# The attention stage of a one-core kernel: output gate through a sigmoid, a reciprocal of eight numbers, heads in two halves of the rows, weight splitting moved from GpSimd to ScalarE and VectorE

## The reference

```python
for t in range(S):                       # S = 768, B = 4, H = 8, D = 40
    m_new = np.maximum(f_gate[:, :, t] + m, i_gate[:, :, t])
    f_stab = np.exp(f_gate[:, :, t] + m - m_new)
    i_stab = np.exp(i_gate[:, :, t] - m_new)
    C = f_stab * C + i_stab * np.einsum('bhd,bhe->bhde', vt, kt)
    n = f_stab * n + i_stab * kt
    h_tilde = np.einsum('bhde,bhe->bhd', C, qt)
    denom = np.maximum(np.abs(nq), 1.0)  # nq = n . q
    o = 1.0 / (1.0 + np.exp(-o_gate[:, :, t]))
    y[:, :, t] = o * h_tilde / denom
...
x = experts(x, w_gate, w1, w2)           # each token to one expert, relu between w1 and w2
return (x @ w_a) * (x @ w_b) @ w_out     # w_a, w_b: 320 x 1536
```

## Time and profile before

| | |
|---|---|
| median of three runs | 985.36 us (981.37 to 985.89) |
| the profiled execution | 981.72 us, of which 980.0 us are the span |
| attention, first `prob` to last `prob` | 28.37 to 195.76 us |
| of which tiles 3 to 23 | 54.74 to 195.76 us |
| first instruction of `experts` | 209.80 us |
| mean granted TensorE clock | 0.949 |

### The profile page before, as it was taken

How to read it: one execution, slowest core, us unless ns; L and a number is a source line. 1 busy time by engine, 2 the same in 40 slices (tenths; PEclk the granted TensorE clock), 3 DMA queues, 4 the chain that set the end, 5 groups by cost and what they waited for, 6 DMA issues and landing times.

```text
span 980.0 us, 17872 instructions
## 1 busy us (share of the span) xinstructions
PE 854.5 (87%) x6122; PEld 809.0 (83%) x6122; DVE 650.0 (66%) x1639; ACT 257.3 (26%) x493; POOL 187.9 (19%) x218
## 2 busy tenths in 40 slices
PE   1899999943479979998999899899989998999995
PEld 1899899932378979997898799789978988998995
DVE  7489999975756775577558656855775575265222
ACT  5222222200223331232124123312331242233221
POOL 7466767710100110011001100110110011011001
PEclk9989999965689999999999999999999999999998
DMA  3866667200321220041013001200310040032000
GB/s 88 225 170 186 191 186 212 88 13 11 98 71 41 69 77 14 2 119 41 0 31 107 20 0 59 79 20 0 103 56 0 2 135 21 1 93 67 1 1 21
DMA packets 49722, 66.59 MB, mean 68 GB/s; under 512 B 6592, under 2 KB 43984, under 8 KB 48720
## 3 DMA queue, kind: packets, MB, share of 16 engines
q1 hardware_dynamic: 43856, 54.25, 19.4%
q0 software_dynamic: 2368, 7.88, 2.8%
q10 hardware_dynamic: 3456, 3.93, 1.2%
HBM read 57.88 MB, written 8.16 MB: 67 GB/s over the span
## 4 chain that ended last, share of the span: by engine, by line
PE 46%; DVE 20%; issue 5%; ACT 4%; DMA 1%; POOL 1%; DVEq 0%; ACTq 0%; POOLq 0%
PE psA L875 17%; PE acc L898 11%; PE psB L875 8%; PE acc L923 6%; DVE at_slot L1241 2%; DVE ab L1327 2%; DVE w_lo L1265 2%; ACT ab_hi L1075 2%; DVE w_lo L1261 2%; PE psT L935 2%; DMA xg<-xs_dram,idx_g 1%; DVE w_hi L1263 1%; DVE cmp L1103 1%; PE psT L949 1%; PE psT L943 1%
## 5 line engine op out<-in xcount | busy, mean ns | idle before, releaser
L875 PE MATMUL psA<-x_hi,wa 128*128 128x384 f32 x480 | 135.5, 347 | 0.4 <-DVE x_lo L1353 0.4
L875 PE MATMUL psB<-x_hi,wb 128*128 128x384 f32 x480 | 132.3, 341 | 0.0
L840 POOL DMA_INDIRECT xg<-xs_dram,idx_g x24 | 25.6, 1068 | 499.2 <-DVE idx_g L1255 494.3
L875 PE MATMUL psB<-x_lo,wb 128*128 128x384 f32 x288 | 97.0, 337 | 0.0
L875 PE MATMUL psA<-x_lo,wa 128*128 128x384 f32 x288 | 96.9, 336 | 0.0
L1080 ACT COPY a_sb<-psA 128x384 f32<-128x384 f32 x96 | 46.1, 480 | 188.8 <-PE psB L875 188.7
L923 PE MATMUL acc<-wo_hi,ab_hi 128*128 128x320 f32 x288 | 91.9, 319 | 1.0 <-DVE ab_lo L1331 1.0
L923 PE MATMUL acc<-wo_lo,ab_hi 128*128 128x320 f32 x288 | 88.8, 308 | 0.0
L923 PE MATMUL acc<-wo_hi,ab_lo 128*128 128x320 f32 x288 | 88.7, 308 | 0.0
L1331 DVE TENSOR_TENSOR ab_lo<-ab,ab_hi 128x384 fp32r<-128x384 f32 x96 | 53.5, 558 | 52.3 <-ACT ab_hi L1075 52.1
L1327 DVE TENSOR_TENSOR ab<-a_sb,psB 128x384 f32<-128x384 f32 x96 | 52.9, 551 | 52.4 <-ACT a_sb L1080 52.1
(11 more groups left out here) (233 smaller groups left out, 1917.3 us busy)
## 6 DMA issues: line engine op xcount, KB each, us to landing
toks<-in_tok_dram SPq DMA_DIRECT2D x24, 484.0 KB, 5.1
w_raw<-in_w_dram SPq DMA_DIRECT2D x32, 320.0 KB, 3.2
w_raw<-in_w_dram SPq DMA_DIRECT2D x32, 256.0 KB, 3.0
qks<-in_qk_dram SPq DMA_DIRECT2D x24, 320.0 KB
w_raw<-in_w_dram SPq DMA_DIRECT2D x64, 64.0 KB, 2.8
xs_dram<-y ACTq DMA_DIRECT2D x24, 160.0 KB, 3.8
qst<-in_qk_dram SPq DMA_DIRECT2D x48, 60.0 KB
piece<-in_w_a_dram SPq DMA_DIRECT2D x6, 256.0 KB, 2.7
```

The source lines that it names most:

```text
L840: pool.indirect_dma_start(out=xg[:, t, 0:DM], out_offset=None, in_=xrows, in_offset=bass.IndirectOffsetOnAxis(ap=idx_g[:, t:t + 1], axis=0 ...
L875: last = pe.matmul(ps, w, x, start=(n == 0), stop=(n == len(steps) - 1))
```

## The change

1. The gate. `o_gate` is no longer a part of each tile's `toks`; one DMA per chunk (`load_gates`) brings it for four tiles into `gate`, and ACT turns it into a sigmoid in place (`open_gates`, 128x1280), one chunk ahead, in tile 3 of the chunk. Exp and Sigmoid are in different ACT tables, so a table load stands ahead of the sigmoid, and a one-number Exp (`reload`) with another table load behind it. The `ez` of each tile is gone.
2. The reciprocal. DVE takes it of `den` (128x8) right behind `den`. `normalize` multiplies `num` with it (128x320), `finish` multiplies with the gate (128x320).
3. Row halves. Heads 0 to 3 are in partitions 0 to 39, heads 4 to 7 in partitions 64 to 103 of `qks`, `arow` and `mrow`, and `exponents` and `scores` take them in turn: each product is over 40 partitions at 0 or at 64. The `qks` loads are two DMAs rather than one, the `arow`/`mrow` loads four rather than two. `exponents` stands directly behind `scores`, ahead of `transposes`.
4. `transposes` and `logits` take three full blocks of 128 (`y` has 64 more columns, zero).
5. The splitting. `w_a` and `w_b` have loads, semaphores and splits of their own: `load_piece(c, 0)` in SP's queue behind tile 1, `load_piece(c, 1)` behind tile 3. ACT makes the high part (`split_high`, one 128x768 copy) in tiles 0 and 2, DVE the low parts (`split_low`, 128x512 and 64x256) in tiles 1 and 3. POOL has no part in it any more.
6. ACT no longer zeroes `qks` at the start; POOL's memsets have half the columns, and there are eight of six partitions rather than four.

```diff
     def _(sp):
+        def load_gates(c):
+            sp.dma_start(gate[:, bass.ds(c, 1), :, :].rearrange("p c b n -> p (c b) n"),
+                         tok[bass.ds(c, 1), :, :, TOK:TOK + DM].rearrange("c b t n -> t (c b) n")).then_inc(sm["og_in"], 16)
...
-                sp.dma_start(qks[b][0:D, :, :, :], qk[bass.ds(c, 1), b].rearrange("c d a h t -> (c d) a h t")).then_inc(qk_in[b], 16)
+                for z in range(2):
+                    sp.dma_start(qks[b][z * HALF:z * HALF + D, :, :, :],
+                                 qk[bass.ds(c, 1), b, :, :, z * HH:(z + 1) * HH, :].rearrange("c d a h t -> (c d) a h t")
+                                 ).then_inc(qk_in[b], 16)
...
+                if b == 1:
+                    load_piece(c, 0)
+
+            load_piece(c, 1)
+            if not (isinstance(c, int) and c == C - 1):
+                load_gates(c + 1)
...
     def _(act):
+        def open_gates(c):
+            act.wait_ge(sm["og_in"], 16 * (c + 1))
+            g = gate[:, bass.ds(c, 1), :, :].rearrange("p c b n -> p (c b n)")
+            act.activation(g, g, ACT.Sigmoid).then_inc(sm["gate_ready"], 1)
+
+        def split_high(c, i):
+            act.wait_ge(sm[f"piece_in{i}"], 48 * (c + 1))
+            act.copy(second[i][:, 0:3, bass.ds(c * FB, FB)], piece[:, i, :, :]).then_inc(sm[f"piece_hi{i}"], 1)
...
                 act.activation(decay[n][:, :, :], psE[:, :, :], ACT.Exp).then_inc(sm["exp_done"], 1)
+                if b % 2 == 0:
+                    split_high(c, b // 2)
+                if b == 3 and not (isinstance(c, int) and c == C - 1):
+                    open_gates(c + 1)
+                    act.wait_ge(sm["y_zero"], 3)
+                    act.activation(reload[:, :], reload[:, :], ACT.Exp, scale=0.0).then_inc(sm["reloaded"], 1)
...
-                act.activation(ez[n][:, :], og(b), ACT.Exp, scale=-1.0).then_inc(sm["ez_ready"], 1)
...
     def _(pe):
-            for h in range(H):
-                last = pe.matmul(psS[:, h, :], qks[b][:, 1, h, :], qks[b][:, 0, h, :], start=True, stop=True)
+            for h in range(HH):
+                for z in range(2):
+                    rows = slice(z * HALF, z * HALF + D)
+                    last = pe.matmul(psS[:, z * HH + h, :], qks[b][rows, 1, h, :], qks[b][rows, 0, h, :], start=True, stop=True)
...
                 if not last_one:
                     scores(u + 1, *nxt)
+                if not last_two:
+                    exponents(u + 2, *after)
                 if not first:
                     transposes(u - 1, 1 - n)
...
     def _(dve):
-            dve.scalar_tensor_tensor(out=zd.rearrange("p (h d) -> p h d", h=H),
-                                     in0=ez[n][:, :].rearrange("p (h d) -> p h d", h=H), scalar=1.0,
-                                     in1=den[n][:, :].unsqueeze(2).broadcast_to([P, H, D]), op0=ALU.add, op1=ALU.mult
-                                     ).then_inc(sm["z_done"], 1)
-            dve.wait_ge(sm["z_done"], v + 1)
-            dve.reciprocal(zr, zd).then_inc(sm["r_done"], 1)
...
+            dve.tensor_tensor(scaled.rearrange("p (h d) -> p h d", h=H), num[n][:, :, 0:D],
+                              rden[n][:, :].unsqueeze(2).broadcast_to([P, H, D]), ALU.mult).then_inc(sm["scale_done"], 1)
...
+            dve.tensor_tensor(y[n][:, 0:DM], scaled, gate[:, bass.ds(cb[0], 1), cb[1], :].rearrange("p c n -> p (c n)"), ALU.mult
+                              ).then_inc(sm["y_ready"], 1)
...
+        def split_low(c, i):
+            w, cols = second[i], bass.ds(c * FB, FB)
+            dve.wait_ge(sm[f"piece_hi{i}"], c + 1)
+            dve.tensor_tensor(w[:, 3:5, cols], piece[:, i, 0:2, :], w[:, 0:2, cols].bitcast(F32), ALU.subtract).then_inc(sm[f"piece_lo{i}"], 1)
+            dve.tensor_tensor(w[64:P, 2, cols], piece[64:P, i, 2, :], w[64:P, 2, cols].bitcast(F32), ALU.subtract).then_inc(sm[f"piece_lo{i}"], 1)
...
+                if b % 2:
+                    split_low(c, b // 2)
...
+                dve.reciprocal(rden[n][:, :], den[n][:, :]).then_inc(sm["r_done"], 1)
```

More of the change, by code:

```diff
@@ L125, in attention @@
     st_old = [sb(f"st_old{n}", [DG, H, DA]) for n in range(2)]
-    ez = [sb(f"ez{n}", [P, DM]) for n in range(2)]
-    y = [sb(f"y{n}", [P, DM]) for n in range(2)]
+    gate = sb("gate", [P, C, B, DM])
+    reload = sb("reload", [P, 1])
+    y = [sb(f"y{n}", [P, DMP]) for n in range(2)]
     xt = [sb(f"xt{n}", [P, 3, P]) for n in range(2)]
@@ L132, in attention @@
     den = [sb(f"den{n}", [P, H]) for n in range(2)]
-    zd = work[0][:, 0:DM]
-    zr = zd
+    rden = [sb(f"rden{n}", [P, H]) for n in range(2)]
+    scaled = work[0][:, 0:DM]
     piece = sb("piece", [P, 2, 3, F2 // C])
@@ L318, in _ @@
             new_state(u)
-            split(c, b)
+        for i in range(2):
+            pool.wait_ge(sm[f"piece_lo{i}"], 2 * C)
         pool.iota(rowi, [[P, C], [S, B]], base=0, channel_multiplier=1).then_inc(sm["made"], 1)
@@ L414, in transposes @@
             at_least(pe, sm["l_copied"], v)
-            for k, (at, w) in enumerate(KS):
-                last = pe.transpose(oT[0:w, k, :], y[n][:, at:at + w], identf[:, :])
+            for k in range(3):
+                last = pe.transpose(oT[:, k, :], y[n][:, k * P:(k + 1) * P], identf[:, :])
             last.then_inc(sm["t_ready"], 1)
@@ L420, in logits @@
             pe.wait_ge(sm["xt_copied"], v + 1)
-            for k, (at, w) in enumerate(KS):
-                last = pe.matmul(oL, xt[n][0:w, k, :], wg[0:w, k, :], start=(k == 0), stop=(k == 2))
+            for k in range(3):
+                last = pe.matmul(oL, xt[n][:, k, :], wg[:, k, :], start=(k == 0), stop=(k == 2))
             last.then_inc(sm["l_ready"], 1)
@@ L426, in _ @@
         scores(0, 0, 0)
+        exponents(1, 0, 1)
         def chunk(c):
@@ L484, in _ @@
         dve.memset(diag[:, :, :], 1.0).then_inc(sm["wg_zero"], 1)
+        dve.memset(reload[:, :], 0.0).then_inc(sm["y_zero"], 1)
+        for n in range(2):
+            dve.memset(y[n][:, DM:], 0.0).then_inc(sm["y_zero"], 1)
+        for b in range(B):
+            dve.memset(toks[b][:, TOK:], 0.0).then_inc(sm["y_zero"], 1)
         dve.wait_ge(sm["wg_zero"], 4)
```

131 lines of the change are left out of this document (55 added, 76 removed).

## The result

The changed kernel took 986.78 us as the median of 20 runs (983.2 to 992.26), the kernel before 982.55 us in 20 runs beside it (979.0 to 985.89). The ratio is 1.0045, with a 95% interval of 1.0031 to 1.0059: slightly slower. The prediction said 951 us and gave 0.93 to faster.

A forecast was written before the change was run, and what follows sets the result against it. VectorE was taken as the bound, TensorE 0.4 us behind; afterwards TensorE at 5.97 us a tile. Gains of 21.6 (middle tiles), 5.9 (first tiles) and 3.0 (tail) sum to 30.5, taking 981.72 to 951 us; range 942 to 973.

The forecast's parts named there:

- several small waits taking it back: Whole kernel: rival of no effect to speak of, small waits cancelling the gain; chance 0.02.
- The first tiles and the last: Attention's tiles 0 to 2 in 20.5 us, 5.9 won; behind the last `prob`, 3.0 us won.
- The price of two halves in turn: TensorE's `psS`: halves load weights in parallel, 1.0 us instead of 1.87; setting changes cost 2 x 0.16; chance 0.60.
- weight loads serial: TensorE's halves in attention: rival that loads follow each other, 6.84 us a tile, 971 us in all; chance 0.22.
- position change: TensorE: rival that going from partitions 0 to 64 costs like a setting change, about 1029 us; chance 0.04.
- TensorE becomes the bound at 5.97 us: Attention tiles 3 to 23: period falls from 7.05 to 5.97 us, 21.6 us won over 20 periods.
- SP issues three more DMAs a tile, and its loads lead by some three tiles. I cost it at nothing: SP's DMA queue in attention: the extra DMAs are covered by the loads' lead, cost zero.
- were that cover gone, `exponents` would wait for `row_in`: Attention: if SP's loads lost their lead, `exponents` would wait for its rows; no size of its own.
- The same size if the loads of rows come late: Attention: late row loads cost 7 us, 958 in all; chance 0.12 shared with the rival of late table switches.
- VectorE at 4.9 us a tile: Attention tiles 3 to 23: VectorE's work falls to 97.7 us, 4.9 a tile, no longer the bound.
- ScalarE's switches: Tile 3 of each chunk: 4.0 us hidden with 0.5 to spare; rival that they are late, 958 us, chance 0.12.
- `experts` is the same code: The stage after attention: unchanged code, predicted difference 0.

The follow-up runs named there:

- a_zouter: Changed kernel with `psS`'s four heads of partitions 0 to 39 first, then those of 64 to 103, instead of in turn; 986.45 us.
- a_both_shift: Changed kernel with q and k laid out by the host for one run per row, piece loads on ScalarE's queue, and 77 empty VectorE instructions; 957.48 us.
- a_both_lowpool: a_both_shift with the 64x256 low parts on GpSimd instead of VectorE, fillers keeping the loop of turns in place; 942.72 us.
- a_shift77: Changed kernel with 77 empty VectorE instructions spread over the eight written-out tiles of attention, ahead of the loop of `experts`; 971.33 us, ratio 0.9901 to the kernel before.
- a_both_zouter: a_both_shift with the two halves of `psS` one behind the other instead of in turn; 953.15 us.

## Why the prediction was wrong

The time fell within 0.5% of before, for which I had one case at 0.02, "several small waits taking it back". It was two large terms.

- **The first tiles and the last: near in number.** 20.65 us predicted as 20.5, and the tail gave 4.4 us rather than 3.0. No wait of GpSimd for a piece, no low clock in tiles 0 to 2. That the 20.5 was so close is luck in part: I had three equal tiles and 2.6 us of waits, and the tiles took 8.9, 6.6 and 5.2 us, with ScalarE waiting 4.3 and 3.9 us for its pieces. The 2.4 us ahead of the first `prob` I had not looked at, and no run here tells where they come from.
- **The price of two halves in turn: right.** `psS` 0.97 us for 1.0. The changes of setting too: from the start of `psO` to that of `psS` it is 1.96 us where it was 1.78, 0.18 for the 0.16 that I took. TensorE's tile is 5.53 us where I had 5.97. By the starts, 0.23 of the difference is `psE` with the change behind it (0.43 for 0.50 + 0.16), 0.11 `psS`, 0.08 the logits. The rivals "weight loads serial" and "position change" are out. Here the Trainium skill (TensorEngine Tiling (Array Packing), Theoretical Speedup), up to twice as fast, held: 1.87 to 0.97 us for `psS`, of which the order of the halves gives 0.55 (a_zouter).
- **"TensorE becomes the bound at 5.97 us": this is the first step that failed**, by the sentence "SP issues three more DMAs a tile, and its loads lead by some three tiles. I cost it at nothing". I had counted the DMAs and not their price, and the profile of before held the price of everything but the 2 KB runs. SyncE needed 7.1 us a tile, without a wait of its own. The condition that I wrote beside it, "were that cover gone, `exponents` would wait for `row_in`", is what happened (eight waits, 13.8 us). The -21.6 us became -0.3.
- **"The same size if the loads of rows come late", 7 us: mis-sized.** Late rows also meant late pieces (43.8 us of ScalarE's waits) and toks (9.0 us of GpSimd's), and a clock of 0.93 over the stage.
- **VectorE at 4.9 us a tile: mis-sized.** It is 113.7 / 20 = 5.7, and 6.0 in the version without waits (a_both_shift). I priced `y` as if it kept its length, and it went from 12.0 to 17.2 us in the window; `den` took 6.2 for 3.4. The low parts I priced at 0.689 + 0.422, 11.1 us, from a stage in which GpSimd does little, and they took 18.3. Beside GpSimd the small one costs 0.85 to 0.99. "VectorE stops being the bound" held only until SyncE was mended.
- **ScalarE's switches: right in the changed kernel, and part of a wait of 1.2 us a chunk in a_both_lowpool.** The rows at 100 us have a table load of 1.28, the sigmoid 1.27, a load of 1.28 and the short Exp 0.20, with nothing between them. The Trainium skill (ScalarE: Activation LUTs, What ACT_TABLE_LOAD costs) would add 1.38 us to each load. No run here shows it: the first load starts 0.02 us behind the end of `decay`. At 5.5 us a tile, and with a piece's DMAs in the same queue, the 0.5 us of slack are gone, and `copy_xt` and then the logits are late, in the order that the prediction gave.
- **"`experts` is the same code": the second step that failed.** The stage that I took as unchanged was 18.4 us longer. 15.4 of them are the same code at another place of VectorE's program: at the end of each of four turns VectorE stands idle for 2.6 us and TensorE for 5.4, with the low clock behind. The other 3 us are in turns that vary by as much from run to run. With the loop resident the changed kernel was 15 us faster and 1% faster than before (a_shift77).

With both failures mended the time is 957.5 us, 6 over the predicted 951, and VectorE is the bound again. Only with the 64x256 parts on GpSimd as well does it come to 942.7 us. That is another kernel than the one priced, so it does not make the number right; it shows that the mechanism on TensorE was. What stood in its way was SyncE's queue and the fetches, on which the sum had no term, and then VectorE, priced too low.

## What to carry to other kernels

Before pricing a change on the engines that compute, add up what each DMA queue issues per tile, by its rows in the timeline, with the number of contiguous runs of each DMA: a queue that was idle half the time can become the bound when loads are cut in two. If it never waits, it is the bound. Durations taken from a stage in which the neighbour engine is idle are the lower end of a range. And when a later, untouched stage gets slower, look turn by turn, at the instruction queues and at idle time marked "issue" behind a loop's back edge; a few empty instructions ahead of the loop test that in one run.

## What the runs showed of the hardware

- VectorE's instructions come in packets of 8 KB, and a hardware loop of 325 records a turn costs 5 or 6 packets in each turn or none to one, by its place: resident with 77, 96 and 108 fillers, not with 0, 48, 60 and 128. Over four turns it is worth 11 to 18 us. The Trainium skill (Runtime: NRT & Kernel Launch, Instruction fetch mechanics) has the room for instructions as two lines of 16 KB; by that, places 128 instructions apart need not be alike. Here 0 and 128 were alike, both fetched, with resident places between them. The page's warning, that a taken branch out of the window costs a fetch, the rows bear out.
- Issuing one DMA of 160 KB over 40 rows takes SyncE 0.4 us with runs of 4 KB and 0.8 to 0.9 with runs of 2 KB; 320 KB in 40 runs of 8 KB took 0.30. For the three DMAs of a piece GpSimd needs 0.74, 0.55 and 0.52 us where SyncE needs 0.41, 0.55 and 0.53.
- Sixteen f32 weight loads of 128 columns over 40 partitions take 0.97 us when two places in the rows alternate and 1.52 when they do not; over 96 partitions it was 1.87.
- VectorE's operations on eight numbers, 0.17 us alone, take up to 1.0 us beside GpSimd's, and end with them (a_both_shift).
- A version with a longer `psS` was 4 us faster (a_both_zouter), with the clock at 1.00 instead of 0.97.
